# Delta-rule attention fused with a first expert layer: attention steps re-spaced on TensorE, the inverse taken in three parts, one bank not lent in two tiles

## The reference

```python
def _attn_ref(q, k, v, beta):                       # 4 x 8 heads, 768 steps, 48 wide
    k_n = k / (np.linalg.norm(k, axis=-1, keepdims=True) + 1e-06)
    state = np.zeros((B, H, D, D))
    for t in range(S):
        y[:, :, t] = einsum('bhd,bhde->bhe', q[:, :, t], state)
        v_old = einsum('bhde,bhd->bhe', state, kt)
        state = state + bt * einsum('bhd,bhe->bhde', kt, vt - v_old)
# then, with x = y as 3072 tokens x 384:
h = x @ w_in;  x = (max(h, 0) + log1p(exp(-|h|))) @ w_out      # first layer, 2048 hidden
h = x @ w_in2; x = (h * cos(h)) @ w_out2                       # second layer
```

## Time and profile before

| | us |
|---|---|
| median of 3 runs (1006.55 to 1009.58) | 1007.16 |
| the profiled execution | 1011.04 |
| its span, first to last instruction | 1009.2 |
| PE busy in it | 967.7 |
| DVE, ACT, POOL busy | 728.6, 517.0, 331.8 |
| mean granted TensorE clock | 0.973 |

### The profile page before, as it was taken

The page is one execution under the profiler, slowest core; times in us unless marked ns, Lnnn a source line. Parts: engine busy times, 40 slices in busy tenths (PEclk is TensorE's granted clock), DMA queues, the critical chain, the costliest instruction groups (busy, mean ns, idle before and its releaser), DMA issues.

```text
span 1009.2 us, 24453 instructions
## 1 busy us (share of the span) xinstructions
PE 967.7 (96%) x10472; PEld 807.4 (80%) x10472; DVE 728.6 (72%) x1122; ACT 517.0 (51%) x848; POOL 331.8 (33%) x417
## 2 busy tenths in 40 slices
PE   4879899999999999999999999999999999999998
PEld 3777687888788787888788888888888888888897
DVE  4978875878586868765645677877868778688775
ACT  3565653663546365445635535545555455454543
POOL 2079738802960494079000695100101001001000
PEclk9569999999999999999999999999999999999999
DMA  9304113102110220011005321000101002010011
GB/s 213 61 20 110 32 50 65 48 1 48 36 48 18 50 63 2 19 34 48 1 18 165 118 63 63 1 0 15 48 1 35 29 7 57 0 28 5 1 32 32
DMA packets 110683, 42.57 MB, mean 42 GB/s; under 512 B 89040, under 2 KB 105936, under 8 KB 110576
## 3 DMA queue, kind: packets, MB, share of 16 engines
q1 hardware_dynamic: 105984, 39.73, 15.8%
q10 hardware_dynamic: 4592, 1.28, 0.7%
HBM read 31.56 MB, written 9.44 MB: 41 GB/s over the span
## 4 chain that ended last, share of the span: by engine, by line
PE 73%; POOL 14%; DVE 8%; issue 3%; ACT 1%; DMA 0%; SPq 0%; DVEq 0%; POOLq 0%
PE wide L1811 11%; PE bank L1811 9%; POOL inv L553 7%; PE wide L1789 7%; PE wide L1790 7%; PE wide L1791 7%; POOL blk L550 6%; PE wide L1818 5%; PE bank L1818 4%; PE bank L1791 4%; PE bank L1790 4%; PE bank L1789 4%; DVE blk L1002 1%; PE bank L1357 1%; DVE inv L1103 1%
## 5 line engine op out<-in xcount | busy, mean ns | idle before, releaser
L1789 PE MATMUL wide<-x_hi,wi_hi 128*128 128x512 f32 x408 | 162.8, 399 | 4.7 <-DVE inv L1133 3.3
L1310 DVE TENSOR_TENSOR g_lo<-tmp,g_hi 128x512 fp32r<-128x512 f32 x192 | 154.5, 805 | 6.6
L1790 PE MATMUL wide<-x_lo,wi_hi 128*128 128x512 f32 x408 | 159.1, 390 | 0.0
L1791 PE MATMUL wide<-x_hi,wi_lo 128*128 128x512 f32 x408 | 159.0, 390 | 0.0
L909 ACT ACTIVATE tmp<-wide 128x512 f32<-128x512 f32 x88 | 52.7, 598 | 162.2 <-PE wide L1791 157.7
L553 POOL TENSOR_TENSOR inv<-inv,blk 128x31 f32<-128x31 f32 (+15 forms) x155 | 116.8, 753 | 12.1
L1811 PE MATMUL wide<-g_hi,wo_hi 128*128 128x512 f32 x304 | 119.8, 394 | 0.5 <-issue 0.5
L1811 PE MATMUL wide<-g_hi,wo_lo 128*128 128x512 f32 x304 | 119.7, 394 | 0.0
L590 POOL TENSOR_TENSOR x_lo<-x_raw,x_hi 128x1536 fp32r<-128x1536 f32 x6 | 23.2, 3862 | 269.2 <-ACT x_hi L622 269.2
L1308 DVE CAST g_hi<-tmp 128x512 fp32r<-128x512 f32 x192 | 96.3, 502 | 19.9 <-DVE tmp L1301 0.5
L1291 DVE TENSOR_SCALAR tmp<-tmp 128x512 f32<-128x512 f32 x96 | 54.5, 568 | 73.5 <-ACT tmp L900 73.5
(11 more groups left out here) (196 smaller groups left out, 1963.5 us busy)
## 6 DMA issues: line engine op xcount, KB each, us to landing
stage<-in_moe_w_in SPq DMA_DIRECT2D x32, 192.0 KB, 3.4
stage<-in_moe_w_out SPq DMA_DIRECT2D x8, 768.0 KB, 5.2
qn<-in_q SPq DMA_DIRECT2D x24, 192.0 KB, 4.0
x_t<-x_res SPq DMA_DIRECT2D x6, 768.0 KB, 3.4
x_raw<-x_t SPq DMA_DIRECT2D x6, 768.0 KB, 4.9
res_v<-in_v SPq DMA_DIRECT2D x22, 192.0 KB
out_x<-res SPq DMA_DIRECT2D x160, 24.0 KB, 1.5
kn<-in_k SPq DMA_DIRECT2D x32, 96.0 KB, 3.0
```

What stands on the lines that cost most here:

```text
L1310: nc.vector.tensor_tensor(lo, g, hi.bitcast(FP32), ALU.subtract).then_inc(g_ready, 1)
L1789: mm(dst, wi_hi[:, ft, kt, :], hi[:, kt, :], start=(kt == 0), stop=False)
L1790: mm(dst, wi_hi[:, ft, kt, :], lo[:, kt, :], start=False, stop=False)
L1791: last = mm(dst, wi_lo[:, ft, kt, :], hi[:, kt, :], start=False, stop=(kt == KT - 1))
```

## The change

- On PE, DVE and ACT the pieces of places 20 to 28 move. Now: KS1 20, Y0 21, V1 22, Q1 23, SN1 and P1 24, YT0 25, Y1 26, YT1 27, KS0 of the next chunk 28.
- The first half of Y1 is lent an h bank too (26), and KS0 is lent at 28. M1 is no longer lent in chunks 1 and 5; both halves go to spare banks.
- `take_inverse` is split into `turn_solved` (the transpose, with the wait for POOL) and `scale_inverse`. In chunks 2 to 4 DVE does turn_solved at place 8, scale_inverse 9, turn_inverse 10, take_inner 12 and 13 (before: both at 7, turn_inverse 9, take_inner 12 and 13). In chunk 5: turn_solved and scale_inverse 9, turn_inverse 11, both take_inner 13. In chunk 1 only the functions' names change.
- `take_blocks` of the four blocks: at places 17, 19, 19, 20 (before 19, 19, 21, 21).
- ACT's first `fill_diagonal` moves behind T0.

```diff
-LENT = {"P0": 4, "M1": 12, "V0": 16, "SN0": 18, "KS1": 20, "V1": 22, "SN1": 24}
-LENT_AHEAD = {"KS0": 26}
+LENT = {"P0": 4, "M1": 12, "V0": 16, "SN0": 18, "KS1": 20, "V1": 22, "SN1": 24, "Y1": 26}
+LENT_AHEAD = {"KS0": 28}
...
-            elif _job in LENT and (_c, _job) != (1, "P0"):
+            elif _job in LENT and (_c, _job) not in ((1, "P0"), (1, "M1"), (NCH - 1, "M1")):
...
-            take_inverse(c)
-            yield
-            yield
-            turn_inverse(c)
-            yield
-            yield
-            yield
-            take_inner(c, 0)
-            yield
+            yield
+            if after:
+                turn_solved(c)
+            yield
+            if not after:
+                turn_solved(c)
+            scale_inverse(c)
+            yield
+            if after:
+                turn_inverse(c)
+            yield
+            if not after:
+                turn_inverse(c)
+            yield
+            if after:
+                take_inner(c, 0)
+            yield
+            if not after:
+                take_inner(c, 0)
             take_inner(c, 1)
...
             if after:
                 take_s(c + 1, 0, "S0")
+                take_blocks(c + 1, 0)
             yield
             take_state(c, 0, "SN0")
             yield
             if after:
-                take_blocks(c + 1, 0)
                 take_blocks(c + 1, 1)
+                take_blocks(c + 1, 2)
             yield
             take_rest(c, 1, "KS1")
-            yield
             if after:
-                take_blocks(c + 1, 2)
                 take_blocks(c + 1, 3)
...
             keys_on_state(c, 1, "KS1")
+            yield
             read_out(c, 0, "Y0")
+            yield
+            solve_values(c, 1, "V1")
             yield
             pe.wait_ge(q_loaded, 64 * c + 64)
             transposes(c, "Q1", qn)
             yield
-            solve_values(c, 1, "V1")
+            add_to_state(c, 1, "SN1")
             scores(c, 1)
             yield
-            yield
-            add_to_state(c, 1, "SN1")
-            yield
             turn_out(c, "YT0", "Y0")
+            yield
+            read_out(c, 1, "Y1")
+            yield
+            turn_out(c, "YT1", "Y1")
             yield
             if after:
                 keys_on_state(c + 1, 0, "KS0")
-            read_out(c, 1, "Y1")
-            yield
-            turn_out(c, "YT1", "Y1")
-            yield
```

More of the change, by code:

```diff
@@ L53 @@
          "V1", "YT0", "S1")
-ORDER_1 = ("Q0", "S0", "KS0", "P0", "T1", "S1", "T0", "M1", "F1", "S0", "V0", "SN0", "KS1", "Y0", "Q1", "V1", "P1", "SN1",
-           "YT0", "KS0", "Y1", "YT1")
-ORDER = ("Q0", "P0", "T1", "S1", "T0", "M1", "F1", "S0", "V0", "SN0", "KS1", "Y0", "Q1", "V1", "P1", "SN1", "YT0", "KS0", "Y1",
-         "YT1")
+ORDER_1 = ("Q0", "S0", "KS0", "P0", "T1", "S1", "T0", "M1", "F1", "S0", "V0", "SN0", "KS1", "Y0", "V1", "Q1", "SN1", "P1",
+           "YT0", "Y1", "YT1", "KS0")
+ORDER = ("Q0", "P0", "T1", "S1", "T0", "M1", "F1", "S0", "V0", "SN0", "KS1", "Y0", "V1", "Q1", "SN1", "P1", "YT0", "Y1", "YT1",
+         "KS0")
 LENT_1 = {"KS0": 4}
-LENT = {"P0": 4, "M1": 12, "V0": 16, "SN0": 18, "KS1": 20, "V1": 22, "SN1": 24}
-LENT_AHEAD = {"KS0": 26}
+LENT = {"P0": 4, "M1": 12, "V0": 16, "SN0": 18, "KS1": 20, "V1": 22, "SN1": 24, "Y1": 26}
+LENT_AHEAD = {"KS0": 28}
 CONTENT = {}
@@ L863, in attention @@
                 take_transposes(c + 1, "T0", knT[:, fill_of(c + 1, 0)])
+                fill_diagonal(c, 1)
             yield
             yield
+            if not after:
+                fill_diagonal(c, 1)
             fill_diagonal(c, 0)
@@ L1114, in begin, with turn_solved, scale_inverse @@
             first_solve()
[L1116 removed]
+        def turn_solved(c):
             dve.wait_ge(inv_ready, c + 1)
             nc.vector.transpose(invN.rearrange("p u c -> p c u"), inv[:, :, :].rearrange("p i c -> p c i")).then_inc(invN_step, 1)
+        def scale_inverse(c):
             dve.wait_ge(invN_step, c + 1)
@@ L1142, in first @@
         def first():
-            take_inverse(0)
+            turn_solved(0)
+            scale_inverse(0)
             turn_inverse(0)
@@ L1171, in attention_1 @@
             yield
+            scale_keys(2)
             take_p(1, "P0")
-            scale_keys(2)
             yield
@@ L1178, in attention_1 @@
             yield
-            take_inverse(1)
+            turn_solved(1)
+            scale_inverse(1)
             yield
@@ L1192, in attention_1 @@
             take_s(2, 0, "S0")
+            take_blocks(2, 0)
             yield
@@ L1195, in attention_1 @@
             yield
-            take_blocks(2, 0)
             take_blocks(2, 1)
+            take_blocks(2, 2)
             yield
             take_rest(1, 1, "KS1")
+            take_blocks(2, 3)
             yield
-            take_blocks(2, 2)
-            take_blocks(2, 3)
             yield
@@ L1205, in attention_1 @@
             yield
-            take_p(1, "P1")
             yield
             take_state(1, 1, "SN1")
+            take_p(1, "P1")
             yield
@@ L1211, in attention_1 @@
             yield
-            take_rest(2, 0, "KS0")
             yield
@@ L1215, in attention_1 @@
             yield
+            take_rest(2, 0, "KS0")
             yield
@@ L1258, in attention @@
             if after:
-                take_blocks(c + 1, 0)
                 take_blocks(c + 1, 1)
+                take_blocks(c + 1, 2)
             yield
             take_rest(c, 1, "KS1")
+            if after:
+                take_blocks(c + 1, 3)
             yield
-            if after:
-                take_blocks(c + 1, 2)
-                take_blocks(c + 1, 3)
             yield
@@ L1269, in attention @@
             yield
-            take_p(c, "P1")
             yield
             take_state(c, 1, "SN1")
+            take_p(c, "P1")
             yield
@@ L1275, in attention @@
             yield
-            if after:
-                take_rest(c + 1, 0, "KS0")
             yield
@@ L1280, in attention @@
             yield
+            if after:
+                take_rest(c + 1, 0, "KS0")
             yield
@@ L1683, in attention_1 @@
             yield
-            solve_values(1, 1, "V1")
+            add_to_state(1, 1, "SN1")
             scores(1, 1)
-            yield
-            yield
-            add_to_state(1, 1, "SN1")
             yield
@@ L1691, in attention_1 @@
             yield
-            keys_on_state(2, 0, "KS0")
             read_out(1, 1, "Y1")
@@ L1696, in attention_1 @@
             yield
+            keys_on_state(2, 0, "KS0")
             yield
@@ L1752, in attention @@
             yield
-            if after:
-                keys_on_state(c + 1, 0, "KS0")
             read_out(c, 1, "Y1")
@@ L1758, in attention @@
             yield
+            if after:
+                keys_on_state(c + 1, 0, "KS0")
             yield
```

3 lines of the change are left out of this document (1 added, 2 removed).

## The result

| | before | after |
|---|---|---|
| median of 7 runs each, us | 1009.0 (1006.55 to 1010.73) | 1002.4 (999.06 to 1004.41) |
| the profiled execution, us | 1011.04 | 1003.1 |
| its span, us | 1009.2 | 1001.2 |

The changed kernel takes 0.9934 of the time before, 95% interval 0.9915 to 0.9952: 6.6 us faster. The forecast was 11.6 less. It was made from the first three runs of before (median 1007.16); with more runs before stands nearer to 1009. From profiled execution to profiled execution the gain is 7.9.

What follows compares the result with a forecast made beforehand. PE, busy nearly all the time, was held bound by stops for missing instructions and waits for take_inner and g_hi. Gains 8.7 + 2.5 + 0.85 + 2.2 less 2.6 make 11.6 us: 1007.16 to 995.6, range 991.5 to 1002.5.

Steps and rivals of the forecast that it cites:

- Part 1: KS and Y set apart on PE: stops for missing instructions go in chunks 1 to 4, gaining 8.7 us.
- rival (1): Loads of v, q, k still starve PE; if chunks 1 and 2 keep their losses, 1002.5 us; chance 0.13.
- the islands' cost: More groups of small matmuls between products on PE, chunks 1 to 5, at 0.23 us each: 2.6 us lost in all.
- Part 3: Inverse parted, blocks earlier: waits behind POOL go, gaining 0.85 us in chunk 4 and 2.2 in chunk 5.
- the cover: Earlier blocks put POOL in time by 1.7 us; with their old order it would be 1.7 late.
- Part 2: M1 not lent in chunk 1: product1's 3.30 us wait for take_inner goes, gaining 2.5 us, bounds 0 and 3.4.
- a sign of being wrong: DVE waiting at L1120 was listed among what would show the forecast wrong; no size given.
- a long stop costs twice: Behind PE's long stops in chunks 1 and 2 the clock averages 0.55 and 0.66 of 2.4 GHz for 3.8 to 4.1 us.
- rival (2): Bank and inverse gains only move to waits at F1 or next g_hi, chunks 1 and 5: 1000.3 us; chance 0.17.
- DVE's margin: Behind KS1's start, product2 of slice 11 needs g_hi at 9.0 us, DVE gives it at 7.8: 1.2 us of room.
- rival (3): DVE late at the fourth block, product2 of slice 11 waits in chunks 1 to 4: up to 1009.6 us; chance 0.05.

Runs made afterwards that it cites:

- part1_only: Kernel before with only outputs and keys on state set apart on PE; blocks, inverse and banks nearly all as before: 1007.96 us, ratio 0.9990 to before.
- part1_blocks: Kernel before with KS and Y set apart and the four blocks at their new places; inverse places and bank as before: 1005.05 us, ratio 0.9939 to before.
- m1_lent_c1: Changed kernel with M1 of chunk 1 again written into a lent bank: 1005.64 us, ratio 0.9966 to the kernel before.
- block3_late: Changed kernel with the fourth block of the inverse one place later, behind main of slice 11: 999.51 us, ratio 0.9904 to the kernel before.
- fill_f1: Changed kernel with ten overwritten products put on PE ahead of F1 of chunk 1: 1002.06 us, ratio 0.9929 to the kernel before.
- parts 2 and 3 alone: Kernel before with M1 not lent, inverse split and blocks at their new places, PE's attention steps as before: 1005.52 us, ratio 0.9954 to before.

## Why the prediction was half right

**What held.** The sign. Part 1: the stops went in all chunks, with the loads where they are, so rival (1) is out. KS1 to KS1 was forecast at 90.9 us and is 90.86 and 90.88 from chunk 2 on, which bears out the gain less the islands' cost; the first, from chunk 1 to 2, is 92.19. Part 3: the waits for GpSimd of chunks 4 and 5 went, F1 in chunk 5 waits 1.3 (forecast 1.4), and both stretches came out within 0.02. That the early blocks are the cover without which a faster PE gains nothing was shown by part1_only and part1_blocks.

**Part 2's sum failed in its last step.** "So PE reaches F1 early, waits there some 1 us, and 2.5 of 3.4 remain." F1 came as forecast. But PE came 1.8 us earlier to chunk 1's S1, 0.9 by the new order of `scale_keys`, which the prediction had left out, and 0.9 by an earlier start of the chunk. The time of F1 stayed, since POOL's end sets it: a wait of DVE for POOL of 1.80 us at L1120, which the prediction had named as a sign of being wrong. So the wait at F1 was 2.2, and I charged nothing for the clock behind it, though the prediction itself says that a long stop costs twice. That was 3.0 us in this profile. In chunk 1 rival (2) thus came true in the profile, by the clock more than by the wait; in chunk 5 it did not. Against m1_lent_c1, where the clock falls too, the term is right.

**DVE's margin failed by one term.** The fourth block was put 6.6 us behind KS1's start; it ended at 241.89, 6.5 behind 235.38. Its g_hi was put at 7.8, with 1.2 of room. The copy would have ended at 7.8 with its usual 0.43, and ended at 9.3. The prediction went through the queues of the moved steps, but GpSimd's scaling, which the fourth block releases, was moved as well, onto the copy that PE needs next. 0.2 us idle in each of chunks 2 to 4, more in chunk 1: about 1 us in the row of chunk 1, 1.7 in all by the windows of block3_late. That is rival (3)'s place, by another mechanism, at a price too small to turn the sign.

**The starting point.** 1007.16 was the low end of what before shows (1008.6 to 1011.2 in later groups). It took 1.8 us off the forecast time. The measured 1002.4 lies just inside the range. Of the forecast gain of 11.6, 7.9 came from profile to profile and 6.6 from median to median. The 3.7 between the first two are the two terms above. The 1.3 between the last two is no more than where each profiled execution lies, 2.0 above the median of before and 0.7 above that of the change. How the 3.7 divide in the unprofiled executions stays open, since fill_f1, which took the slow clock away in its profile, was no faster.

**What the parts are worth** (us, from the medians of each group): part 1 0.7; part 1 with the blocks 6.1; parts 2 and 3 alone 4.2; all 6.6. Part 1 and parts 2 and 3 alone make 4.9, 1.7 less than all together, which the intervals don't resolve. What they do resolve is part 1 with and without the early blocks: PE goes at the pace of the later of its instructions and the inverse, and with the stops gone DVE's waits for POOL grew from 2.4 to 6.2 us until the blocks were moved. The early blocks without parts 1 and 2 were not run, so what they are worth by themselves is open.

## What to carry to other kernels

When a step is moved, list what it releases on other engines too: an operation of GpSimd that now starts beside a VectorE copy can hold that copy until it has ended; cutting it up or starting it one step later took PE's wait away here and cost little. When PE is made faster ahead of a wait whose time another engine sets, only the wait grows, and the clock behind it can fall, as it did in ten of eleven profiles here; a few products thrown away there kept the clock up in two profiles here, with a gain in time that is likely in one kernel and absent in the other. Test the parts alone and in pairs: one that shows nothing alone may be what lets the other work.
